# One Trainium2 core: the last layer's first product by block products in quads, with value tiles between, and gates ahead of the last value tiles

## The reference, cut to what matters

```python
xk = mu_k * x + (1.0 - mu_k) * x_prev        # x_prev: x of the token before
xr = mu_r * x + (1.0 - mu_r) * x_prev
k = np.maximum(xk @ w_k, 0.0)                # w_k 512 x 1024
v = k * k @ w_v                              # w_v 1024 x 512
r = 1.0 / (1.0 + np.exp(-(xr @ w_r)))        # w_r 512 x 512, the gate
return (r * v).astype(np.float32)
```

## Time and profile before

| | us |
|---|---|
| median of 3 runs (lowest, highest) | 487.44 (486.76, 487.47) |
| the profiled execution, its own time | 486.72 |
| its span, first to last instruction | 485.0 |
| PE busy | 465.2 |
| DVE busy | 298.6 |
| ACT busy | 227.4 |
| POOL busy | 149.9 |

### The profile page before, as it was taken

The page is one execution under the profiler, slowest core; times in us unless marked ns, Lnnn a source line. Parts: engine busy times, 40 slices in busy tenths (PEclk is TensorE's granted clock), DMA queues, the critical chain, the costliest instruction groups (busy, mean ns, idle before and its releaser), DMA issues.

```text
span 485.0 us, 7909 instructions
## 1 busy us (share of the span) xinstructions
PE 465.2 (96%) x2896; PEld 418.9 (86%) x2896; DVE 298.6 (62%) x672; ACT 227.4 (47%) x475; POOL 149.9 (31%) x155
## 2 busy tenths in 40 slices
PE   4889899999999999999999999999999999999996
PEld 4777777788999999999999999899899889989985
DVE  6799998487766665447545875666635436354511
ACT  5899997455533234322333332355545325244411
POOL 6656774352236533653216643000000000000000
PEclk9999999999999999999999999999999999999999
DMA  5999954410212121212112315410010010001001
GB/s 164 265 223 236 210 125 71 131 43 1 88 45 70 61 86 45 88 46 85 43 69 63 131 43 174 126 49 1 0 65 1 0 43 22 0 1 64 0 0 65
DMA packets 42235, 36.92 MB, mean 76 GB/s; under 512 B 20704, under 2 KB 34528, under 8 KB 42208
## 3 DMA queue, kind: packets, MB, share of 16 engines
q1 hardware_dynamic: 42208, 36.58, 28.4%
...
## 4 chain that ended last, share of the span: by engine, by line
PE 80%; ACT 7%; issue 5%; DVE 3%; DMA 2%; POOL 2%; SPq 0%; ACTq 0%; POOLq 0%; DVEq 0%
PE bank L1238 19%; PE bank L1240 19%; PE bank L1239 19%; PE bank L1371 13%; PE bank L1372 7%; ACT e_sb L646 4%; DMA v<-in_v_dram 2%; ACT qbd L626 2%; PE bank L1218 1%; PE bank L1290 1%; POOL xL L557 1%; ACT kt L634 1%; PE bank L1308 1%; POOL v L499 1%; PE bank L1268 0%
## 5 line engine op out<-in xcount | busy, mean ns | idle before, releaser
L1238 PE MATMUL bank<-ucH,w1H 128*128 128x384 f32 x168 | 56.8, 338 | 0.3 <-DVE c L1081 0.2
L1240 PE MATMUL bank<-ucH,w1L 128*128 128x384 f32 x168 | 56.5, 336 | 0.0
L1239 PE MATMUL bank<-ucL,w1H 128*128 128x384 f32 x168 | 56.4, 336 | 0.0
L770 ACT ACTIVATE rH<-c 128x384 fp32r<-128x384 f32 x36 | 18.9, 526 | 69.0 <-DVE c L1081 69.0
L1240 PE MATMUL bank<-xkH,WkL 128*128 128x384 f32 x128 | 43.1, 337 | 0.0
L1238 PE MATMUL bank<-xkH,WkH 128*128 128x384 f32 x128 | 43.0, 336 | 0.0
L1239 PE MATMUL bank<-xkL,WkH 128*128 128x384 f32 x128 | 43.0, 336 | 0.0
L1157 DVE SCALAR_TENSOR_TENSOR k<-bank,kr 128x384 f32<-128x384 f32 x32 | 17.8, 556 | 33.4 <-ACT kr L820 33.4
L1240 PE MATMUL bank<-WvH,k2L 128*128 128x512 f32 x96 | 37.8, 394 | 0.0
L598 POOL TENSOR_TENSOR w2L<-stg,w2H 128x512 fp32r<-128x512 f32 x24 | 37.5, 1585 | 1.0
L1239 PE MATMUL bank<-WvL,k2H 128*128 128x512 f32 x96 | 37.8, 394 | 0.0
...
## 6 DMA issues: line engine op xcount, KB each, us to landing
stg<-in_moe_w_ch_dram SPq DMA_DIRECT2D x24, 512.0 KB, 3.4
...
stg<-in_moe_w_k_dram SPq DMA_DIRECT2D x4, 512.0 KB, 3.5
stg<-in_moe_w_v_dram SPq DMA_DIRECT2D x4, 512.0 KB, 4.2
```

What stands on the lines that cost most here:

```text
L770: act.activation(rH[slot][:, f, half * GR:half * GR + GR], src, ACT.Relu).then_inc(rh_done, 1)
L1238: pe.matmul(dst, wH, mH, start=start, stop=False, **more)
L1239: pe.matmul(dst, wH, mL, start=False, stop=False, **more)
L1240: return pe.matmul(dst, wL, mH, start=False, stop=stop, **more)
```

## The change

xk @ w_k is formed like the channel mixing, in eight quads numbered on from 12 to 19 (`NA = NQ + B * NKP`; `NKP` = 4 for each batch), with w_k in w_ch1's place and w_v in w_ch2's. `set_of(q)` is the set of seven combinations that a quad uses: 0 and 1 of u, 2 and 3 of xk of batch 0 and 1. A quad of the last layer (`quad_k` on ACT and DVE) forms the same five sums; DVE squares each result block (`kr * kr`, or max(c, 0) * c), ACT copies the high part and DVE subtracts. Between the products PE places twelve value tiles of the quad before, 3 matmuls of 512 columns each, one tile of 128 tokens in each of banks 2 to 7. Work for a later set stands in tables by quad and place: `mix_k`, `combine_u`, high and low parts, and xr's pieces. Places of `quad_k` on DVE: 1 ahead of P7's sum, 2 ahead of R22's low half, 3 at the end. The second batch's `wide` and `side` move into quad 12, which on PE still has the chunks of quad 11 between its products. w_r is loaded, split (high on ACT, low on POOL) in quad 16, between the pieces of w_v. The six gates of batch 0 come behind quad 16 and its value tiles of quad 15, the outputs of batch 0 with them; the six gates of batch 1 come behind quad 19, and then the value tiles of quad 19 in token order, each followed by DVE's product and a store.

```diff
-        U_AHEAD = ((), (0,), (1,), (3,), (4, 5), (6, 2))
-        T_AHEAD = ((), (3,), (4,), (5,), (6,), ())
-        MIXED_AFTER = {NQ - 3: (0, 1), NQ - 2: (2, 3), NQ - 1: (4,)}
-        LAST_QUAD = {NFP + 2: LAST_ORDER[0], NFP + 3: LAST_ORDER[1], NFP + 4: LAST_ORDER[2]}
...
+        T_AT = {(1, 0): (3,), (2, 0): (4,), (3, 0): (5,), (4, 0): (6,),
+                (9, 1): (3, 4), (9, 2): (5, 6), (14, 1): (3, 4), (14, 2): (5, 6)}
...
+                (10, 1): (0, 1), (10, 2): (3,), (11, 1): (4, 5), (11, 2): (6, 2),
+                (14, 3): (0, 1), (15, 1): (3, 4), (15, 2): (5, 6), (15, 3): (2,)}
+        MIX_AT = {(7, 1): ((0, 0), (1, 0)), (7, 2): ((2, 0), (3, 0)), (8, 1): ((0, 1), (1, 1)), (8, 2): ((2, 1), (3, 1)),
+                  (13, 1): ((0, 0), (1, 0), (2, 0), (3, 0)), (13, 2): ((0, 1), (1, 1), (2, 1), (3, 1))}
...
+        XR_LOW_AT = {(16, 3): (0, 1, 2, 3), (17, 3): (0, 1, 2, 3), (18, 3): (4, 5, 6, 7)}
+        SLOT2 = [("w2", n) for n in range(16)] + [("wr", 0), ("wr", 1)] + [("w2", n) for n in range(16, NA)]
...
+            def quad_k(q):
...
+                plus(P6, u2, Bk, p1)
+                dve.wait_ge(kr_done, k + 1)
+                dve.tensor_tensor(kr[:, :], kr[:, :], kr[:, :], ALU.mult).then_inc(sq_done, 1)
+                ahead(q, 1)
+                if q == NQ:
+                    wide(1, 0)
+                plus(P7, u3, Bk, p1)
+                low_k(R11, 0, 0, kr)
+                if q < NA - 1:
+                    low_w1(q + 1, 0)
...
+                plus(P5, c22, A, u3)
+                square(R22, c22)
+                ahead(q, 2)
+                if q == NQ:
+                    wide(1, 1)
+                low_k(R22, 1, 1, c22)
+                plus(P4, c21, Bk, p1)
+                square(R21, c21)
+                if q < NA - 1:
+                    low_w1(q + 1, 1)
+                low_k(R21, 1, 0, c21)
+                if q == NQ:
+                    side(1, 1)
+                plus(P3, c12, A, u2)
+                square(R12, c12)
+                low_k(R12, 0, 1, c12)
...
+                ahead(q, 3)
...
+            def gate(b):
+                wait_piece(pe, "wr", 1)
+                for st in range(NT):
+                    if st < 2:
+                        pe.wait_ge(sum_done, 5 * (NQ + NKP + 1 if b == 0 else NA))
+                    else:
+                        pe.wait_ge(sg_done, NT * b + st - 1)
+                    if st % RT == 0:
+                        pe.wait_ge(xrl_done, 8 * b + KT * (st // RT + 1))
...
+            TILE_GAPS = (range(0, 2), range(2, 3), range(3, 5), range(5, 6), range(6, 8), range(8, 10), range(10, 12))
+            for q in range(NA):
                 for n in range(NPROD):
                     product(q, n)
-                    for m in GAPS[n]:
-                        if q:
-                            second(q - 1, *CHUNKS[m])
...
+                    if q > NQ:
+                        for m in TILE_GAPS[n]:
+                            value(q - 1, *TILES[m])
...
+                if q == NQ + NKP:
+                    gate(0)
+            gate(1)
+            for st in range(NT):
+                for f in (1, 0):
+                    value(NA - 1, f, st)
```

More of the change, by code:

```diff
@@ L765, in quad, with ahead @@
+            def ahead(q, place):
+                for kk, half in MIX_AT.get((q, place), ()):
+                    mix_k(set_ahead(q) - B, kk, half)
+                for i in U_AT.get((q, place), ()):
+                    high_u(set_ahead(q), i)
+                for n in XR_AT.get((q, place), ()):
+                    mix_r(q // 17, n)
+                for n in XR_HIGH_AT.get((q, place), ()):
+                    high_xr(q // 17, n)
             def quad(q):
-                b, slot, done = q // NFP, q % 2, NPROD * q
@@ L767, in quad, with high_r @@
[L767 to L770 removed]
+                slot, done = q % 2, NPROD * q
+                def high_r(n, f, half, src, func=ACT.Relu):
+                    act.activation(rH[slot][:, f, half * GR:half * GR + GR], src, func).then_inc(rh_done, 1)
                 def turn_out(*tiles):
@@ new lines, in ahead @@
+            def ahead(q, place):
+                for kk, half in MIX_AT.get((q, place), ()):
+                    mix_k(set_ahead(q) - B, kk, half)
+                for i in T_AT.get((q, place), ()):
+                    combine_u(set_ahead(q), i)
+                for i in U_AT.get((q, place), ()):
+                    low_u(set_ahead(q), i)
+                for n in XR_AT.get((q, place), ()):
+                    mix_r(q // 17, n)
+                for n in XR_LOW_AT.get((q, place), ()):
+                    low_xr(q // 17, n)
@@ L1180, in _ @@
+            outputs(1)
         @block.tensor
@@ L1437, in _ @@
-            with pe.Fori(0, NGR) as g:
-                last(g)
+                    if q > NQ:
+                        for m in TILE_GAPS[n]:
+                            value(q - 1, *TILES[m])
+                    else:
+                        for m in GAPS[n]:
+                            if q:
+                                second(q - 1, *CHUNKS[m])
+                            else:
+                                token(2 * KT + m)
+                if q == NQ + NKP:
+                    gate(0)
```

548 lines of the change are left out of this document (266 added, 282 removed).

## The result

The change makes the kernel slower: 510.31 us (median of 4 runs, 509.42 to 510.58) against 487.46 (486.76 to 487.91) for the kernel before in the same session, a ratio of 1.0467 (95% interval 1.0449 to 1.0485), or +22.9 us. The forecast was 492.5, +5.

The account below looks back on a forecast made before the run. PE's work was taken to bound the kernel, with PE waiting for DVE in the new quads. Savings of 10.0 us against waits of 15.6 gave net +5.6 and a median of 492.5 us, range 486.5 to 497.5.

Parts of the forecast that it names:

- P4 of q = 12: This product waits 1.5 us for a chunk's addition on DVE, part of quad 12's +4.1 us.
- The saving: On PE: 48 fewer matmuls -8.3 us, old quads' waits gone -1.1, shorter tail -0.6, together -10.0.
- the quad's arithmetic of DVE: Last-layer quad without work ahead: DVE's last sum ends at 15.24 us, PE done at 15.64, 0.25 spare.
- What POOL does to DVE: Late quads: POOL's work slows DVE, priced 2.5 us in all; the skill's lock rule would add some 3 us.
- Gates, 4.2 forecast: Ahead of batch 0's gates: PE waits for xr's low halves while POOL's Wr half slows DVE, +4.2 us (3.2 to 5.5).
- the 3.4 forecast without POOL: Ahead of batch 0's gates: PE starts at 19.0 instead of 15.64 us, 3.4 us.
- comes in time: Quad 16: Wr's second low half on POOL, done at 15.8 us, is not late but slows DVE.
- under the gates: Load and split of w2's piece 16 hidden behind batch 0's gates, priced at nothing; 8 us without that cover.
- q = 12 to 14: PE's waits for DVE in these quads: +4.1, +2.7 and +1.7 us, POOL's slowing included.
- q = 18: Priced with q = 17: mixes exceed the spare time, low halves run beside POOL, +0.5 us (0 to 1.5).
- rival (c): Matmul clock falls in the wait ahead of the gates, costing 2 us, total 494.6; chance 15%.
- top corner: All waits at their upper bounds at once, 22.3 us (+12.3 net); called unlikely and left out of the range.

Follow-up runs that it names:

- e16_best2: Changed kernel with the single gains combined (three squares on ACT, POOL held back, queues reordered) and few operations moved; 484.66 us against 488.12 for the kernel before.
- e8_nothing_ahead: Changed kernel without the mixes, combinations and halves for batch 1 in q = 13 to 15, so part of the output is left out; 498.9 us.
- e3_pool_after_xr: Changed kernel with POOL held, after Wr's second low half, until batch 0's eight low halves of xr are written; 505.45 us.
- e9_split_silent: Changed kernel without POOL's split of the w2 pieces 13 to 19, so part of the output is wrong; 504.76 us.
- e2_pool_after_sum: Changed kernel with POOL's sums of w1 also waiting for DVE's fifth sum of quad n - 2; 506.33 us.
- e7_fill_quads: Changed kernel with 22 useless 128-column matmuls on PE ahead of each of q = 13 to 16, none ahead of the gates; 507.81 us.
- e12_square_alone: Changed kernel with three of the four squares of a new quad on ACT instead of DVE; 503.62 us.

## Why the prediction was wrong

**The sign and the mechanism held.** PE was the bound, and the waits stand where they were announced and have DVE as the releaser: P4 of q = 12 (1.34, forecast 1.5), q = 13 to 16, the first gate. After the last matmul it is 508.4 - 504.8 - 0.4 = 3.2 us, forecast 3.3.

**The saving held.** It can't be read alone, but e16_best2 bears it out within half a us: its quads 8 to 10 take 15.64 to 15.65 us, its later quads and the gates take 0.6 (q = 11), 0.3, 0.1, 0.1 and 6.1 us too much, 7.2, q = 8 began 0.25 later than before, and 7.2 + 0.25 - 10.0 = -2.6; its span is 2.1 shorter. e8_nothing_ahead's 15.68 confirms the quad's arithmetic of DVE.

**The step that failed is "What POOL does to DVE".** I priced POOL at 2.5 us in all, by averages of single stretched operations. The runs show something harder: an operation of DVE whose two inputs lie in SBUF and one of POOL that reads SBUF take turns, and the one that comes second waits for the other's end; one with an input in a bank goes on. The Trainium skill (SBUF — State Buffer, Who interferes with whom) states this lock. I had weighed it at 3 us more; here the trace agrees with the rule (2.37 beside POOL's 2.40, 5.14 against 1.96 with POOL at rest, 0.54 to 0.56 with an input in a bank beside POOL), and the rule was worth more, since the sum has to be made on the rows of POOL that meet DVE's critical stretch:
- *Gates, 4.2 forecast, 9.3 waited.* The square gave +1.8, the low half +0.8, the four xr halves 5.14 - 1.96 = +3.2: 5.8 from three meetings with POOL, where 0.8 was priced; with the 3.4 forecast without POOL that is 9.2. I had written that Wr's second low half "comes in time", which it did, but it is DVE that paid; and I had put piece 16 of w2 "under the gates" at nothing, while POOL took it up at 406.30, in the wait itself. e3_pool_after_xr gives 4.0 of it back.
- *q = 12 to 14*, 8.5 forecast, 10.6 waited. Each seam had w1L at 1.76 and a low half at 1.07, +1.1 together, where I allowed 0.2 to 0.7.
- *q = 18*, 0.5 forecast for two quads, 1.8: four low halves against POOL's sums and split (e9_split_silent takes 1.6 of it away).

With half a us each in q = 9 and 11 (e2_pool_after_sum) I estimate POOL's share at 5.8 + 3.2 + 1.6 + 1.0 = 11.6 us (10.9 if the seams go by the distances in e2_pool_after_sum, 2.5 together) where 2.5 stood. That is 8.4 to 9.1 of the 9.8 by which the rests, 25.4, exceed the 15.6 forecast.

**The clock, rival (c), was too small and in one place only.** I had 2 us at the gates at 15%. There it took 1.9, about as priced. But it fell in q = 13, 14 and 15 as well, at rests of 2.3 to 3.1 us. The sentence on the Trainium skill's rule (TensorE: Matmul & The Clock Gate, What's actually happening) had allowed this for two of the three, and I gave it no term. 6.7 us were lost at the lower level, of which the three falls in the quads cost 2.5 net (e7_fill_quads). What the fall at the gates costs net was not separated.

**Adding terms that share a cause.** The range took the upper ends of the waits, +12.3, as unlikely all at once. But they were not independent: one mechanism, POOL against DVE, had a share in nearly all of them, and the clock fell behind the longer ones. The time came out some 10 us above that top corner (487.44 + 12.3).

**Not seen:** most of the waits came not from too much work but from its order in the queues of DVE, ACT and POOL. With three squares of each quad on ACT (6.7 us alone, e12_square_alone) and otherwise order and places, 25 of 32 us went (e16_best2).
